# Rows of x by products of 64 array rows, in pairs that write two banks

## What is computed

```
p_packed = softmax(p k^T / 8) v        # 8 batches, 8 heads, 32 packs per head
x        = softmax(q p_packed^T / 8) p_packed   # 8*576 = 4608 tokens, 8 heads * 64 = 512 features
expert   = argmax((x/|x|) (e/|e|)^T / tau)      # 8 experts, one for each token
x        = gate * (relu(x w1[expert]) w2[expert])
out      = silu(x w_in) w_out
```

## Time and profile before

| | |
|---|---|
| Median of 3 runs | 1456.26 us (1453.97 to 1456.88) |
| Profiled execution, its own time | 1453.96 us |
| Its span | 1452.2 us |
| PE busy | 1414.0 us, 97% of the span, 9813 instructions |
| DVE busy | 982.0 us, 68% |
| ACT busy | 493.9 us, 34% |
| POOL busy | 565.8 us, 39% |
| The four largest groups of L792 (experts and last stage) | 365.1, 323.8, 246.5 and 242.0 us of PE's busy time |
| DMA | 232.99 MB, 160 GB/s over the span |

### The profile page before, as it was taken

How to read it: one execution, slowest core, us unless ns; L and a number is a source line. 1 busy time by engine, 2 the same in 40 slices (tenths; PEclk the granted TensorE clock), 3 DMA queues, 4 the chain that set the end, 5 groups by cost and what they waited for, 6 DMA issues and landing times. The chain is left out here.

```text
span 1452.2 us, 27808 instructions
## 1 busy us (share of the span) xinstructions
PE 1414.0 (97%) x9813; PEld 1274.6 (88%) x9814; DVE 982.0 (68%) x1382; ACT 493.9 (34%) x749; POOL 565.8 (39%) x466
## 2 busy tenths in 40 slices
PE   7999999999999999999999999999999999999996
PEld 4676688778888888888999999999989999999996
DVE  4888554444444444446888888888898778777783
ACT  3887400330001120203554444444453333333331
POOL 1466708797702870705753333332250111101111
PEclk9999999999999999999999999999999999999998
DMA  9994745786513651514444443443683343333430
GB/s 341 356 355 142 274 131 142 219 267 168 205 48 101 210 201 67 169 43 175 133 139 136 121 125 118 128 130 117 204 265 131 117 144 128 132 130 116 144 116 29
DMA packets 141911, 232.99 MB, mean 160 GB/s; under 512 B 11544, under 2 KB 94872, under 8 KB 134304
## 3 DMA queue, kind: packets, MB, share of 16 engines
q1 hardware_dynamic: 103984, 145.24, 30.4%
q10 hardware_dynamic: 26736, 58.65, 12.2%
q0 software_dynamic: 11136, 28.40, 5.8%
HBM read 144.86 MB, written 87.38 MB: 160 GB/s over the span
## 5 line engine op out<-in xcount | busy, mean ns | idle before, releaser
L792 PE MATMUL ps<-wf,xf 128*128 128x256 f32 x3024 | 365.1, 284 | 4.8 <-DVE xf L1912 4.0
L792 PEld LDWEIGHTS ps<-wf,xf 128*128 128x128 f32 x3024 | 364.5, 193 | 5.4 <-DVE xf L1912 2.8
L792 PE MATMUL ps<-xf,wf 128*128 128x256 f32 x2646 | 323.8, 284 | 0.1
L792 PEld LDWEIGHTS ps<-xf,wf 128*128 128x128 f32 x2646 | 319.1, 192 | 0.3 <-ACT cb L1319 0.3
L792 PE MATMUL ps<-weights,hT 128*128 (+1 forms) x1032 | 246.5, 394 | 0.8 <-DVE hT L1798 0.8
L792 PE MATMUL ps<-weights,xT 128*128 (+1 forms) x1008 | 242.0, 395 | 2.4 <-POOL weights L2054 2.0
L792 PEld LDWEIGHTS ps<-weights,hT 128*128 128x128 f32 x1032 | 190.4, 188 | 39.7 <-issue 1.1
L792 PEld LDWEIGHTS ps<-weights,xT 128*128 128x128 f32 x1008 | 185.7, 188 | 41.4 <-issue 4.5
L1185 ACT CAST weights<-stage 128x1024 fp32r<-128x1024 f32 x56 | 58.0, 1052 | 383.4 <-PE ps L792 284.6
L2054 POOL TENSOR_TENSOR weights<-stage,weights 128x1024 fp32r<-128x1024 f32 x56 | 132.6, 2405 | 132.1 <-ACT weights L1185 132.1
L2201 POOL TENSOR_TENSOR h<-h,sg 128x512 f32<-128x512 f32 x72 | 100.3, 1394 | 188.3 <-ACT sg L1333 188.1
(11 more groups left out here) (233 smaller groups left out, 1755.7 us busy)
## 6 DMA issues: line engine op xcount, KB each, us to landing
g_rows<-h SPq DMA_DIRECT2D x144, 256.0 KB, 2.6
raw<-g_rows SPq DMA_DIRECT2D x36, 1024.0 KB, 4.8
stage<-w ACTq DMA_DIRECT2D x53, 512.0 KB, 3.8
w_forms<-fm ACTq DMA_DIRECT2D x16, 896.0 KB
x_in<-x_rows SPq DMA_DIRECT2D x43, 256.0 KB
y_rows<-y_sb SPq DMA_DIRECT2D x43, 256.0 KB
wf_f<-w_forms SPq DMA_DIRECT2D x11, 896.0 KB, 5.2
q_sb<-qT SPq DMA_DIRECT2D x8, 1152.0 KB
```

Source lines behind the costliest of these rows:

```text
L792: mm = pe.matmul(o, left(a_), right(b_), start=first and n == 0, stop=last and n == 2)
```

## The change

`STORED` gives the place at which each 128 features of x are stored: features 128 to 255 (heads 2 and 3 of group 0) and 256 to 383 (heads 0 and 1 of group 1) change places. `rhs` becomes 272 columns wide, 8 logit columns on either side of the 256. A block of tokens now takes six products of 64 array rows: "up" on partitions 0 to 63, which write bank `lo`, and "dn" on partitions 64 to 127, which write bank `lo + 1`. The two of a pair follow each other: 136 moving columns each, then 8 each, then 128 each. The products with the zero half are gone. Bank `lo` holds the sum over both groups of the logits of rows 0 to 63, bank `lo + 1` that of rows 64 to 127, and DVE adds the two as it did before. For the block of 64 tokens a product of one column in bf16 is put ahead, into a PSUM column that nothing reads. `keep_pl` writes the logits in four copies of 64x8 instead of two of 128x8.

```
-XW = 4 * D + E
+XW = 4 * D + 2 * E
+XB = 4 * D + E
+STORED = (0, 2, 1, 3)
...
         def own(par, g):
-            return rhs[par][g][:, E:XW] if g == 0 else rhs[par][g][:, 0:4 * D]
+            return rhs[par][g][:, E:E + 4 * D]
...
                 lo = row_bank(b, k)
-                for g in range(NG):
-                    mm = pe.matmul(bank[lo + g][0:m, 0:XW], tk_aT[g][:, k * P:k * P + m], rhs[par][g],
-                                   start=True, stop=True)
+                if m < P:
+                    pe.matmul(bank[lo][0:1, XB:XB + 1], ones[:, 0:1], ones[:, 0:1], start=True, stop=True)
+                token = slice(k * P, k * P + m)
+                up_, dn = slice(0, 64), slice(64, P)
+                left, mid, end = slice(0, E), slice(E, E + 2 * D), slice(E + 2 * D, XB)
+                own_0, own_1, lg_1 = slice(0, E + 2 * D), slice(E + 2 * D, XW), slice(XB, XW)
+                for rows, o, at, g, cols, first_, last_ in (
+                        (up_, bank[lo], slice(0, E + 2 * D), 0, own_0, True, False),
+                        (dn, bank[lo + 1], slice(2 * D, XB), 1, own_1, True, False),
+                        (up_, bank[lo], left, 1, left, False, True),
+                        (dn, bank[lo + 1], slice(4 * D, XB), 0, lg_1, False, True),
+                        (up_, bank[lo], end, 1, mid, True, True),
+                        (dn, bank[lo + 1], slice(0, 2 * D), 0, slice(E + 2 * D, XB), True, True)):
+                    mm = pe.matmul(o[0:m, at], tk_aT[g][rows, token], rhs[par][g][rows, cols], start=first_, stop=last_)
                 mm.then_inc(x_done, 1)
...
-                        mm = three(bank[n], lambda a_: xT[:, a_, c, :], lambda b_: w[:, b_, lo:lo + 512],
+                        mm = three(bank[n], lambda a_: xT[:, a_, STORED[c], :], lambda b_: w[:, b_, lo:lo + 512],
...
             def keep_pl(b, par):
                 act.wait_ge(pl_done, b + 1)
-                act.copy(packs_lg(par, 0), bank[2][:, 0:E])
-                act.copy(packs_lg(par, 1), bank[2][:, E:2 * E]).then_inc(pl_kept, 1)
+                for g in range(NG):
+                    lg = bank[2][:, g * E:(g + 1) * E]
+                    act.copy(rhs[par][g][0:64, 0:E], lg[0:64])
+                    kept = act.copy(rhs[par][g][64:P, XB:XW], lg[64:P])
+                kept.then_inc(pl_kept, 1)
...
                 act.copy(x_row[par][0:m, k, :].rearrange("p (g c) -> p g c", g=NG),
-                         ps[0:m, lo:lo + 2, 0:XW]).then_inc(x_kept, 1)
+                         ps[0:m, lo:lo + 2, 0:XB]).then_inc(x_kept, 1)
```

More of the change, by code:

```diff
@@ L368, in own @@
         def own(par, g):
-            return rhs[par][g][:, E:XW] if g == 0 else rhs[par][g][:, 0:4 * D]
-        def packs_lg(par, g):
-            return rhs[par][g][:, 0:E] if g == 0 else rhs[par][g][:, 4 * D:XW]
+            return rhs[par][g][:, E:E + 4 * D]
         def row_bank(b, k):
@@ L869, in half @@
                     lo = c * F + n * 512
-                    mm = three(bank[n], lambda a_: x[:, a_, c, :], lambda b_: w[:, b_, lo:lo + 512], c == 0, c == KD - 1)
+                    mm = three(bank[n], lambda a_: x[:, a_, STORED[c], :], lambda b_: w[:, b_, lo:lo + 512], c == 0, c == KD - 1)
                     yield mm
```

## The result

The changed kernel takes **1460.85 us** (median of 20 runs, 1453.37 to 1468.96); the kernel before took 1454.08 in 20 runs on the same chips (1451.32 to 1456.88). The ratio is 1.0044 [1.003, 1.0058], slower by 6.4 us. Forecast were 1455.0 us and no measurable change. The time lies in the range, but the direction and the size are wrong. The median lies 6.8 us above the before kernel's, and the wide spread above it is new.

What follows compares the result with a forecast made beforehand. Attention's batch was taken as bound by a PE loop with ACT holds, then a second loop through DVE and `diagonal`. -1.44 + 0.30 - 0.13 = -1.3 us on 1456.26 gave 1455.0 us; range 1451 to 1466.

Steps and rivals of the forecast that it cites:

- a change of shape: On PE, between products of different array shape: 0.094 us each, plus the open first load (0.107 or 0.057 us).
- the sum: Whole kernel: -1.44 us in six batches, +0.30 in batch 7, -0.13 in the tail, together -1.3 us.
- The PE loop: A batch's chain through all five blocks on PE, with holds by ACT: to gain 0.42 us by itself.
- the loop through `diagonal`: Batch loop over block 1, `logits_packs`, ACT, DVE and `diagonal` to `turn_values` and `scores_packs`: 0.45 us of slack.
- The forecast's base: Starting time: the median of the kernel before, 1456.26 us, from which -1.3 us gave 1455.0.
- halves that take turns: Rival, blocks on PE: a block's 12 instructions stream one after another, 1.00 us; whole kernel 1465 us; 15%.
- The copies' term: ACT, behind `logits_packs`: two more logit copies at 0.06 us each, +0.12 us before `exp_tokens`.
- the second loop: Batch loop through ACT, DVE and `diagonal`: takes 0.21 us of its 0.45 slack, so a batch gains only 0.24 us.
- the forecast's 1.44 less: The six batches ahead of batch 7: 0.24 us gained in each, 1.44 us in all.
- the forecast's +0.30: Batch 7, no pack work on PE: block 0, two shape changes at block 1 and the copies add 0.30 us.
- The tail's term: Tail after the last batch: block 1 gets shorter, then ACT's own pace holds from 144.00; -0.13 us.
- The clock: Rival, PE's clock: one more half-clock stretch like that of the first 30 us costs 3.3 us, giving 1458.3; 8%.

Runs made afterwards that it cites:

- e2: Changed kernel with two logit copies of 128 partitions, each writing both places, instead of four: 1456.79 us, ratio to before 1.0019.
- e1: Kernel before with four logit copies of 64x8 instead of two of 128x8, products unchanged: 1458.26 us against 1454.78, ratio 1.0025.
- e4: Kernel before with each 128-row product of a block cut to 136 columns, result not the reference's: 1449.9 us, ratio 0.9961.
- t4: Kernel before with the tail's products each cut into three column pieces, 12 instructions a block: tail 13.39 us, against 10.86 before.
- u2: Kernel before with the tail's products each cut into two column pieces, 8 instructions a block: tail 13.66 us, against 10.86 before.
- s: Constants at PE's start cut into 40, 80 or 120 pieces in e2, tails 14.00, 14.04, 13.69 us; into 80 in the kernel before, tail 11.09.
- a2: Changed kernel run again unaltered, with a second profile: 1461.40 us in six runs, ratio to before 1.0062.
- u1: e2 with the tail's blocks in two products of 264 columns, 4 instructions each, result not the reference's: 1454.4 us, ratio 0.9998.
- e3: Changed kernel with two products of constants ahead of block 3 in each batch: 1458.24 us, ratio to before 1.0032.
- e7: e2 with constant products between the tail's blocks, behind each batch's second `turn_packs`, and before the last batch's block 3: ratio to before 1.0026.

## Why the prediction was wrong

**What held.** The loop of a batch and the block. 12 instructions end to end in 0.95 us (0.94 forecast), the halves at once, 0.09 us at a change of shape. Inside the block two errors cancel: in each half the second 8-column instruction starts 0.03 us behind the first, where the sum charged 0.11 since it "can't be shorter than a weight load", and the second of 128 columns 0.19 behind the first, where it charged 0.11. The Trainium skill's "TensorE: Matmul & The Clock Gate", Part 3, says that products on different row groups overlap; the trace agrees, two of a pair start 0.007 us apart. The PE loop was said to gain 0.42 us by itself, and with the copies' cost out (e2) a batch gains 0.42. That the numbers agree is luck: in e2 it is the loop through `diagonal` that holds the batch, and for it the slack of 0.45 less 0.03 and 0.06 gives 0.36. DVE and `diagonal` came next, as said, but in e2 only; in the changed kernel `scores_packs` is released by ACT as before. Behind attention PE has the same 8779 instructions, and the stage took 1299.6 and 1301.3 us, within the 1298.5 to 1302.9 of the six profiles of before and its variants (before, e1, e4, t4, u2, s). a2's excess over before's 1298.5 is not time at half clock, of which it has less there, 13.2 us against 14.3.

The forecast's base was off too. The -1.3 us were laid on a median of three runs, 1456.26; twenty gave 1454.08. And that 1460.85 lies in the range is luck: the range reached there for halves that take turns, and they do not.

**The copies' term was mis-sized.** "Two more logit copies at 0.06 us each", +0.12 on the second loop. Four copies take 0.70 us to `exp_tokens` where two took 0.12, so +0.58. The row behind the price was of copies over 128 partitions; that of a half was taken to be the same. The term stands in both loops, and it is the PE loop that shows it. Block 3 starts 4.04 us behind block 1 in a2 and 3.69 before, +0.35 where the sum had -0.17. From there to `turn_packs` it is -0.28, as in the sum, and block 0 adds its 0.03: the batch is 15.43 at full clock and not 15.1, a loss of 0.10 where -0.24 was forecast. Beside the copies the sum let ACT's copy of block 2 follow `exp_tokens` after 0.59 us; it follows after 0.71. The way from batch 0 to 6 takes 1.1 us more at full clock for the forecast's 1.44 less. Of these, 0.7 are in the last one (14.64 us for 13.95), which is the one that the forecast's +0.30 was nearest to.

**The tail's term had the wrong sign.** -0.13, with the reason that ACT's own pace holds from 144.00. Measured: +2.5 in a2 and e2, with the blocks at half clock, and +2.5 and +2.8 in t4 and u2, at full clock in the kernel before. t4, u2 and u1 show it to go with more than 4 PE instructions in a block of the tail. The step counted the block's stream and nothing else. In the changed kernel's own first profile the idle time does not appear, and the tail took 12.27 us, 1.4 more than before. The half clock of its blocks is no reason for that, since a2, e2 and e3 had it and the idle time too.

**The clock was the rival that came true, and it was mis-sized.** It had 8% and one more stretch like that of the first 30 us, at 3.3 us. What spoke against it was the batch's mean share of PE, 14.79 of 15.32. What fell was the share in one place: 2.90 of 3.40 us behind block 1, where it was 3.26. That was the work of the late copies as much as of the lighter blocks: e1, with the old blocks, has 2.90 in that place too. And 2.90 is no sign by itself, since a2 has 2.89 there in the same batches with the clock up. The price of one was right in kind: a batch with one is longer by 1.60 us (17.03 - 15.43), 1.97 in e7, 1.87 in u1. Their number was not: the work repeats in each batch, and so may the fall. Six stretches make 6 x 1.6 = 9.6 us in the profiled run, none in a2.

**The sum.** Taken out one after the other by edits, the costs are these. The copies: 1.0044 (1.0062 in a2) falls to 1.0019 in e2, 3.6 or 6.3 us, the lost time in the loop and most of its falls. The instructions of the tail's blocks: 1.0019 falls to 0.9998 in u1, 3.1 us. By the clock the same loss reads otherwise: of the 13.3 us that the mean run has more at half clock, 6.8 would be the tail's, if each run has it as both profiles do, and the other 6.5 two falls in the loop, 3.1 us of time. With 1.1 us for the copies and 1.4 to 2.5 for the tail that makes 5.6 to 6.7 of the 6.4 us; it is an estimate. It also says that the 5.4 us of the line hold part of the copies and the tail. Not explained are the four fastest runs, 1453.4 to 1454.8 us: they leave no room over before for 1.1 + 2.5.

**Open.** What delays PE's signals in the tail is not known, only that it comes with 8, 12 or 16 instructions in the blocks there and not with 4, whatever their rows. Nor is it known whether the 0.4 us in single batches of the loop have the same cause; they are seen only in kernels with two copies and pairs. Why one execution falls in each batch and the next in none is not known either: nothing in the kernel differs. e3's filling on top of e2's two copies was not tried in its place before block 3. A version with the pairs in the loop, 4 instructions a block in the tail and the right order of x was not tried.

## What to carry to other kernels

Where PE is busy 0.96 of a loop, a saving there can be taken back by PE's own clock. Look for the wait of PE that a change creates (here 0.50 us before block 3) and not at the mean share, and multiply a stretch at half clock by the number of times that the loop passes it. Price a small copy by a row with its own partitions: here two copies over 128 partitions, each into both places, take 0.6 us less than four of 64. A term goes into every loop that passes it, and the loop with the least slack before it (0.24 us here, not 0.45) sets what it costs. Count what a change adds in instructions as well as in columns in a tail without slack: 8 or 12 in a block instead of 4 cost 2.5 to 2.8 us there, by a mechanism that no busy time shows.

## What the runs showed that was not expected

- Copies of 64x8 on ACT, alternating between the halves of the partitions, start 0.175 us apart; 128x8 and 128x16 ones 0.06 apart.
- Pairs of 64 rows stream at once: 12 instructions of 136, 8 and 128 columns in 0.95 us, against 1.18 for 8 of 128 rows with the same result.
- In one execution the clock was at 1.2 GHz for 3.4 us in each of six batches, in another of the same kernel in none; 1453.4 to 1469.0 us. All ten falls in loops followed a wait of 0.36 to 0.59 us before block 3.
- PE's signals came 1.6 to 5 us after the recorded end of its products, with ACT and DVE idle, in every profiled tail with over 4 instructions a block but one, the kernel before's (t4, u2) among them, at full and at half clock.
